# Router logits of five token groups moved from TensorE to VectorE, in a one-core attention, MLP and mixture-of-experts kernel

## The reference

```python
# attention: q, k, v (4, 8, 576, 64), mask: block of 64 of i >= block of j
x = attn_out.transpose(0, 2, 1, 3).reshape(2304, 512)
gate = 1.0 / (1.0 + np.exp(-(x @ w_gate)))          # w_gate, w_val (512, 1536)
x = (gate * (x @ w_val)) @ w_out                    # w_out (1536, 512)
logits = x @ moe2_w_gate                            # (512, 8)
expert_idx = np.argmax(logits, axis=1)
probs = softmax(logits)                             # denominator + 1e-9
for e in range(8):                                  # w1 (8, 512, 1024), w2 (8, 1024, 512)
    mask = expert_idx == e
    out[mask] = probs[mask, e] * (np.maximum(x[mask] @ w1[e], 0) @ w2[e])
```

## Time and profile before

| | |
|---|---|
| median of 3 runs | 969.89 us (969.75 to 971.04) |
| the profiled execution | 971.46 us, its span from first to last instruction 969.7 us |
| mean granted TensorE clock | 0.987 of full speed |
| TensorE products busy | 914.7 us, 94% of the span |
| VectorE busy | 391.9 us, 40% |
| ScalarE (ACT) busy | 297.2 us, 31% |
| GpSimd (POOL) busy | 260.2 us, 27% |

### The profile page before, as it was taken

How to read it: one execution, slowest core, us unless ns; L and a number is a source line. 1 busy time by engine, 2 the same in 40 slices (tenths; PEclk the granted TensorE clock), 3 DMA queues, 4 the chain that set the end, 5 groups by cost and what they waited for, 6 DMA issues and landing times.

```text
span 969.7 us, 15847 instructions
## 1 busy us (share of the span) xinstructions
PE 914.7 (94%) x5402; PEld 759.7 (78%) x5403; DVE 391.9 (40%) x851; ACT 297.2 (31%) x657; POOL 260.2 (27%) x253
## 2 busy tenths in 40 slices
PE   7988998999999999999999999999887999989995
PEld 3544554589999999999999999999766888878884
DVE  5766776731211321340241153145543345362241
ACT  4554554532221212112122111223132334361140
POOL 4122335421111111111111111122233435462251
PEclk9999999999999999999999999999999999999998
DMA  4545455422200100000010001111045246282130
GB/s 140 158 146 156 155 187 157 138 97 70 73 33 1 33 1 33 4 30 33 1 34 32 1 1 67 44 44 66 33 151 184 98 161 208 80 271 110 43 130 27
DMA packets 45545, 83.18 MB, mean 86 GB/s; under 512 B 6831, under 2 KB 19119, under 8 KB 45488
## 3 DMA queue, kind: packets, MB, share of 16 engines
q1 hardware_dynamic: 39728, 67.21, 21.1%
q0 software_dynamic: 3360, 10.49, 3.2%
q10 hardware_dynamic: 2400, 4.72, 1.3%
HBM read 68.17 MB, written 14.75 MB: 86 GB/s over the span
## 4 chain that ended last, share of the span: by engine, by line
PE 80%; DMA 7%; issue 4%; DVE 3%; POOL 2%; ACT 1%; SPq 1%; POOLq 0%; DVEq 0%; ACTq 0%
PE bank L1388 22%; PE bank L1390 22%; PE bank L1389 22%; DMA rinv_scratch<-rinv 3%; PE bank L1360 3%; PE bank L1321 3%; PE bank L1333 3%; DMA rwide<-rinv_scratch 2%; PE bank L1542 2%; PE bank L1450 2%; POOL w1l L441 1%; DVE nmax L976 1%; PE bank L1441 1%; PE bank L1510 1%; DMA stage<-in_we 1%
## 5 line engine op out<-in xcount | busy, mean ns | idle before, releaser
L1388 PE MATMUL bank<-xh,w1h 128*128 128x384 f32 x576 | 195.3, 339 | 0.0
L1390 PE MATMUL bank<-xh,w1l 128*128 128x384 f32 x576 | 193.0, 335 | 0.0
L1389 PE MATMUL bank<-xl,w1h 128*128 128x384 f32 x576 | 192.8, 335 | 0.0
L686 POOL TENSOR_TENSOR hl<-hraw,hh 128x384 fp32r<-128x384 f32 x72 | 77.6, 1077 | 399.7 <-ACT hh L829 399.7
L1134 DVE TENSOR_TENSOR hraw<-sig,bank 128x384 f32<-128x384 f32 x72 | 39.9, 554 | 269.8 <-ACT sig L873 234.6
L873 ACT ACTIVATE sig<-bank 128x384 f32<-128x384 f32 x72 | 35.4, 492 | 270.3 <-PE bank L1390 270.2
L1388 PEld LDWEIGHTS bank<-xh,w1h 128*128 128x128 f32 x576 | 108.2, 188 | 2.1
L1389 PEld LDWEIGHTS bank<-xl,w1h 128*128 128x128 f32 x576 | 108.2, 188 | 1.4
L1390 PEld LDWEIGHTS bank<-xh,w1l 128*128 128x128 f32 x576 | 108.1, 188 | 0.0
L800 ACT ACTIVATE prob<-bank,nmax 128x576 f32<-128x576 f32 (+2 forms) x144 | 76.0, 529 | 89.0 <-DVE nmax L976 87.9
L1390 PE MATMUL bank<-woh,hl 128*128 128x512 f32 x216 | 85.5, 396 | 0.0
(11 more groups left out here) (202 smaller groups left out, 1370.6 us busy)
## 6 DMA issues: line engine op xcount, KB each, us to landing
stage<-in_we SPq DMA_DIRECT2D x48, 512.0 KB, 4.5
w1raw<-in_w SPq DMA_DIRECT2D x8, 768.0 KB, 4.7
kt<-in_kT SPq DMA_DIRECT2D x16, 288.0 KB, 3.3
qt<-in_qT SPq DMA_DIRECT2D x16, 288.0 KB, 4.1
rwide<-rinv_scratch SPq DMA_DIRECT2D x32, 144.0 KB, 2.9
xt_scratch<-xo SPq DMA_DIRECT2D x16, 288.0 KB, 2.2
xraw<-xt_scratch SPq DMA_DIRECT2D x6, 768.0 KB, 4.6
y_scratch<-yrow ACTq DMA_DIRECT2D x6, 768.0 KB, 3.5
```

Of the source, the lines that this page charges most:

```text
L686: pool.tensor_tensor(hl[:, f % 2, :], hraw[:, f % 2, :], hh[:, f % 2, :].bitcast(F32), ALU.subtract).then_inc(h_low, 1)
L1388: pe.matmul(out_, wh, ah, start=first, stop=False, skip_group_check=True)
L1389: pe.matmul(out_, wh, al, start=False, stop=False, skip_group_check=True)
L1390: return pe.matmul(out_, wl, ah, start=False, stop=last, skip_group_check=True)
```

## The change

The logits of groups 0 to 4 are computed on VectorE: one `tensor_tensor_reduce` for each tile and expert multiplies the 512 values of a row of y with a column of the router's weights and sums them. The weights are spread over all partitions once (`wrb`, 2 MB, the eight experts side by side for each input). They stand in steps 0 to 7, three in each; in the last group 4, 4, 8 and 8 in steps 0 to 3. `routes`, `ranks`, `slots` with `spread`, and `table` follow in steps 8 to 11 (last group: 4 to 7), and the table is added at the next group's step 0. Group 5's own logits stay with TensorE. The ranks take two products instead of six, and the table holds only token numbers (144 columns).

The gates are no longer in the table: a small DMA stores each group's gates as column 513 of `y_dram`, so that a gathered row brings its gate, which GpSimd copies to `wcols` ahead of the next gather.

There is one x buffer: ACT and VectorE split the next group's x in four chunks behind the last `up` of a group, and the last two downs are no longer interleaved with ups of the next. `sig` is gone; the sigmoid is written to `hraw`. The y copies move from step 2 to step 0. The first expert's weights use the four stages of the others, and the steps of their splits are set in tables.

```diff
-    y_dram = nc.dram_tensor("y_scratch", (N, D), F32, kind="Internal").ap()
+    y_dram = nc.dram_tensor("y_scratch", (N, D + 1), F32, kind="Internal").ap()
...
+        def route_steps(G):
+            if G == G_LAST:
+                return [0, 4, 8, 16, 24], 4, 5, 6, 7
+            return [3 * f for f in range(9)], 8, 9, 10, 11
+
+        ROWS0_STEP = 9
+        HIGH_STEP = {6: [0], 7: [1, 2], 8: [3], 9: [4, 5], 10: [6, 7]}
+        LOW_V_STEP = {7: [0], 8: [2], 10: [4, 5], 11: [6]}
+        LOW_POOL_STEP = {8: [1], 9: [3], 11: [7]}
...
+            sp.dma_start(wrb[:].rearrange("p d e -> p (d e)"),
+                         wr.rearrange("(a d) e -> a (d e)", a=1).to_broadcast([P, D * E])).then_inc(wrb_loaded, 16)
+
+            def gate_store(G):
+
+                sp.wait_ge(gates_done, G + 1)
+                sp.dma_start(y_dram[G * GT:(G + 1) * GT, D:D + 1].rearrange("(m p) a -> p m a", p=P),
+                             gate[:].unsqueeze(2), allow_slow_non_contiguous=True).then_inc(gate_stored, 16)
+
             for G in range(2, NG):
                 xload(G, NPAIR)
+                gate_store(G - 2)
...
-                    if isinstance(l, int) and l == 0 and k == 3:
-                        low_wait(sp, l, 0)
+                    if isinstance(l, int) and l == 0 and k == 4:
+                        gate_store(G_LAST - 1)
                     if k >= 4:
-                        low_wait(sp, l, k - 3 if isinstance(l, int) and l == 0 else k - 4)
+                        low_wait(sp, l, k - 4)
...
             sp.wait_ge(first_known, 1)
-            sp.wait_ge(wo_low, FC)
-            sp.wait_ge(x_low, NG)
-            sp.wait_ge(gv_done, FC * G_LAST)
+            sp.wait_ge(lg_out, GM * G_LAST)
             load(0)
+            gate_store(G_LAST)
...
+                    pool.wait_ge(yg_loaded, 16 * t)
+                    pool.tensor_copy(wcols[:, bass.ds(t, 1)], yg[:, D:D + 1]).then_inc(gcol_done, 1)
...
+            def logits_of(G, lo, hi):
+
+                for n in range(lo, hi):
+                    m, e = n // E, n % E
+                    i = GM * G + m
+                    if e == 0:
+                        dve.wait_ge(y_out, i + 1)
+                    steps_done = GM * E * G + n
+                    if steps_done >= 2:
+                        dve.wait_ge(lg_step, steps_done - 1)
+                    junk = yT[:].rearrange("p c n -> p (c n)") if n % 2 else bank[3][:, 1, :]
+                    dve.tensor_tensor_reduce(junk, yrow[:, m, :], wrb[:, :, e], 1.0, 0.0, ALU.mult, ALU.add,
+                                             logits[:, i, e:e + 1]).then_inc(lg_step, 1)
+                    if e == E - 1:
+                        dve.wait_ge(lg_step, steps_done + 1)
+                        dve.sem_inc(lg_out, 1)
...
+                if G != G_LAST:
+                    xhigh(G + 1, [0])
+                hhigh(FC * G + FC - 1, 1)
+                if G != G_LAST:
+                    xhigh(G + 1, range(1, C))
...
-                pe.matmul(rank_psum, ltri_r[:], hot, start=True, stop=False, skip_group_check=True)
-                pe.matmul(rank_psum[:, E:], ones_r[:], hot[:, 0:(GM - 1) * E], start=False, stop=False,
+                pe.matmul(rank_psum, ones_r[:], hots[:, 0:GM + 1, :].rearrange("p m e -> p (m e)"), start=True, stop=False,
                           skip_group_check=True)
-                pe.matmul(rank_psum[:, 2 * E:], ones_r[:], hot[:, 0:E], start=False, stop=True, skip_group_check=True)
+                pe.matmul(rank_psum[:, 0:GM * E].rearrange("p (m e) -> p m e", e=E), ltri_r[:], oneh, start=False, stop=True,
+                          skip_group_check=True).then_inc(ranks_done, 1)
...
                     if f >= 2:
                         down(G, f - 2)
-                    elif not first:
-                        down(G - 1, FC - 2 + f)
...
+                    if not first and f == route_steps(G)[2]:
+                        ranks(G - 1)
+                    if not first and f == route_steps(G)[4]:
+                        table(G - 1)
                     if G == G_LAST and f == ROWS0_STEP:
-                        pe.wait_ge(base_done, G)
+                        pe.wait_ge(table_added, G)
                         turn_rows(0, True)
...
+                down(G, FC - 2)
+                down(G, FC - 1)
```

More of the change, by code:

```diff
@@ L118, in bass_attention_ffn_moe @@
         scol = sb(ctx, "scol", [P, 1], U32)
-        wcol = sb(ctx, "wcol", [P, 1])
-        yg = sb(ctx, "yg", [P, D])
+        wcols = sb(ctx, "wcols", [P, NTAB])
+        sc = ExitStack()
+        ltri = sb(sc, "ltri", [P, P])
+        ones = sb(sc, "ones", [P, P])
+        sc.close()
+        yg = sb(ctx, "yg", [P, D + 1])
         s12 = ExitStack()
@@ L165, in bass_attention_ffn_moe @@
         sx.close()
[L168 to L177, removed]
         sg = ExitStack()
         sb(sg, "over_x", [P, 3 * C * GT])
[L180 to L183, removed]
+        sb(sg, "over_hraw", [P, 2 * GT])
+        yT2 = sb(sg, "yT2", [P, C, P])
+        sb(sg, "over_gates", [P, 4 * GT - C * P + 2 * FC * D])
+        tab = sb(sg, "tab", [P, NCOL])
+        ag = sb(sg, "ag", [P, GM, NCOL], F32R)
+        b1h = sb(sg, "b1h", [P, GM, P], F32R)
+        assert (GM + 1) * NCOL + GM * P <= 2 * D
         sg.close()
@@ L227, in bass_attention_ffn_moe @@
         s3.close()
+        sb(s4, "over_tables", [P, 2 * FC * D - 2 * HC * D + 2 * D])
+        stage = [sb(s4, f"stage{i}", [P, F2]) for i in range(4)]
+        assert 4 * F2 == D * E and HC * P == F2
         s4.close()
@@ L405, in bass_attention_ffn_moe, with stage_at @@
         o_psum = bank[3][:, 0, :]
-        def stage_at(l, k):
-            return stage_first[k % 3][:] if isinstance(l, int) and l == 0 else stage[k % 4][:]
+        def stage_at(k):
+            return stage[k % 4][:]
         def low_wait(eng, l, k):
@@ L475, in bass_attention_ffn_moe @@
         for G in range(NG):
[L476 to L482, removed]
+            SHIFTED.append(n + 2)
+            ONEHOT.append(n + ROUTE_OPS)
+            n += ROUTE_OPS + SLOT_OPS + SPREAD_OPS + (GATE_OPS if G == G_LAST else 0)
+            TABLE.append(n)
+            n += GATE_OPS + 1 + (FIRST_OPS + ROWS_OPS if G == G_FIRST else 0)
         block = ctx.enter_context(nc.Block())
@@ L741, in _ @@
             pool.wait_ge(y_stored, 16 * NG)
+            pool.wait_ge(gate_stored, 16 * NG)
             gather(1)
@@ L871, in group @@
                     if not (first and f < 2):
-                        act.wait_ge(hraw_done, n - 1)
-                    act.activation(sig[:, f % 2, :], gv_psum(f)[0], ACT.Sigmoid).then_inc(sig_done, 1)
+                        act.wait_ge(h_high, n - 1)
+                        act.wait_ge(h_low, n - 1)
+                    act.activation(hraw[:, f % 2, :], gv_psum(f)[0], ACT.Sigmoid).then_inc(sig_done, 1)
                     if first:
@@ L1130, in group @@
                     dve.wait_ge(sig_done, n + 1)
-                    if not (first and f < 2):
-                        dve.wait_ge(h_high, n - 1)
-                        dve.wait_ge(h_low, n - 1)
-                    dve.tensor_tensor(hraw[:, f % 2, :], sig[:, f % 2, :], val_ps, ALU.mult).then_inc(hraw_done, 1)
+                    dve.tensor_tensor(hraw[:, f % 2, :], hraw[:, f % 2, :], val_ps, ALU.mult).then_inc(hraw_done, 1)
                     if first and f == 0:
@@ L1168, in _ @@
             for G in range(NG):
-                group(G, G % 2)
-            weights_low(dve, 0, 0, [k for k in LOW_V if k + EW_STEP + 1 >= FC], ew_low_v)
+                group(G)
             for m in range(GM):
-                yT_evac(GM * (NG - 1) + m, m, last=True)
+                yT_evac(GM * G_LAST + m, m)
             for m in range(GM):
-                lg_evac(GM * (NG - 1) + m, m, last=True)
+                lg_evac(GM * G_LAST + m, m)
             routes(G_LAST)
@@ L1579, in _ @@
             pe.wait_ge(exp_done, NB * NPAIR)
-            up(0, 0, 1)
+            up(0, 1)
             for G in range(NG):
-                group(G, G % 2)
-            down(NG - 1, FC - 2)
-            down(NG - 1, FC - 1)
-            i = GM * (NG - 1)
+                group(G)
             for m in range(GM):
-                turn_y(i + m, m, last=True)
+                turn_y(GM * G_LAST + m, m)
             for m in range(GM):
-                router(i + m, m, last=True)
+                router(m)
             expert_up(0, 0, 0)
             turn_hidden(0)
-            table_last()
+            table(G_LAST)
             expert_down(0, 0, 1)
```

338 lines of the change are left out of this document (137 added, 201 removed).

## The result

In the comparison behind the prediction the changed kernel took 955.32 us (median, 953.58 to 957.25) and the kernel before 970.46 on the same chip: a ratio of 0.984 with a 95% interval of 0.981 to 0.987, or -15.1 us. The forecast was 951.0 with a range of 941 to 961 and 0.92 for faster. The profiled execution has a span of 955.5 us against 969.7, at a mean granted clock of 0.976 against 0.987. So about a fifth of the forecast gain is missing, and most of this part is about where it went.

The account below looks back on a forecast made before the run. TensorE was taken to bound the kernel. From a span of 969.7 us, -27.4 (TensorE's stream), +8.2 (last group), +0.8 (first expert's weights), +0.1 (group 4's end) and -0.8 (tail) gave 950.6, forecast as 951, range 941 to 961.

Parts of the forecast that it names:

- TensorE's stream, -27.4: Groups 0 to 4: removing transposes, router products and their wait from TensorE saves 27.4 us, 26.1 at the other bound.
- The product, 1.05 us: Each new VectorE product of 512 elements, second operand at a 32-byte step, takes 1.05 us; bounds 0.63 and 1.6.
- The slope of L955: Existing VectorE operation reading one SBUF operand at nine floats' step: 1.94 ns an element, used to price the new product.
- contiguous rival: The 32-byte step costs nothing (0.63 us a product), so VectorE is no limit in the last group: 942.6 us; chance 0.24.
- Hidden in groups 1 to 4, and group ends: Products hide under TensorE in groups 1 to 4; splitting the next x at group ends costs nothing, 0.1 in group 4.
- rival of open group ends: At five group ends hl(11) and the x differences delay each other, up 0 waits 1.3 us: 957.5 us; chance 0.10.
- slower one: Products from 1.61 us make groups 1 to 4 wait too: 969.4 us at 1.65, 975 at 1.7; chance 0.06.
- The last group, +8.2: Last group: VectorE needs 36.0 us before the ranks, TensorE 29.3; a 6.7 us stall plus 1.5 for clock adds 8.2.
- The clock term: Last group, after the stall: three microseconds at half the clock (1.2 GHz) cost 1.5 us.
- First expert's weights, +0.8: Last group: late splits of the first expert's weights delay hl(10), so down 10 waits; 0.4 to 2.2 us, taken as 0.8.
- The tail, -0.8: After the last down: fewer rank products and earlier hrow save 1.0, extra gate copies cost 0.25; net -0.8, bounds 0 and -1.6.
- The sum: Whole kernel: 969.7 - 27.4 + 8.2 + 0.8 + 0.1 - 0.8 = 950.6 us of span, a change of -19.1.

Follow-up runs that it names:

- the other layout: Changed kernel with the router's weights laid out expert by expert, so each product reads 512 neighbouring floats: 945.03 us, 0.971 of the kernel before.
- the run with 21 tiles: Changed kernel with group 4's 24 products over only 256 of 512 values, so its tokens go to other experts: 956.57 us, 0.984 of the kernel before.
- the weights in pairs: Changed kernel with the router's weights in pairs of experts, read at a step of two floats instead of eight: 946.48 us, 0.973 of the kernel before.
- the ranks one step later: Changed kernel with ranks, slots and table of the last group in steps 6, 7, 8 instead of 5, 6, 7: 952.11 us, 0.979 of the kernel before.
- the second trace of the changed kernel: The changed kernel run again without any edit, as base beside another experiment: 955.43 us, 0.982 of the kernel before.

## Why the prediction came out as it did

**TensorE's stream, -27.4.** Right. Groups 1 to 3 give 81.2 - 75.65 = 5.55 us each, where 5.45 were forecast (27.4 is five times 5.47, before rounding); group 4 gives 0.5 less for its end, see below, and the fifth sits in the last group.

**The product, 1.05 us.** Right in kind and a little small: 1.09 from start to start. The slope of L955, at a step of nine floats, did carry over to eight. The Trainium skill (VectorE: DVE Perf Modes, Mode 1×) gives fp32 one result a cycle, odd strides included. Beyond a step of two floats the measurement differs from that, and it decides: 683 ns at two, 1,117 at eight. The contiguous rival was a right picture of another kernel: forecast at 942.6, built with the other layout it took 945.0.

**Hidden in groups 1 to 4, and group ends.** Right. No up waits for x or hraw in them; group 4's last step brings hl(11) late, and the sigmoids of step 0 of groups 4 and 5 are 76.18 us apart instead of 75.65: it cost 0.5, where 0.1 was forecast. The rival of open group ends and the slower one fall with this.

**The last group, +8.2.** The place and the mechanism were right (TensorE idle first at up 5, then at the ranks, then at half the clock); the size was short. VectorE's sum was 37.0 us where 36.0 were forecast. Hardly any of that is the product's price: the 24 products and the hl in their midst took 28.35 us, where 25.2 + 3.0 were forecast, since each of the three hl cost 0.73 to 0.85 us instead of 1.0 (0.85 = 1.94 - 1.09), which made up for most of the 0.04 of each product. The excess lies beside them: the table and first_rows with the gap behind them took 2.9 us instead of 2.4, and the five hraw with the gaps ahead of them 3.0 instead of 2.6. TensorE would have been there at 29.0 instead of 29.3: 8.0 us late instead of 6.7. The clock term was 1.5, and is 10.4 - 8.0 = 2.4. I had taken three microseconds at the low clock, the length of the stretch of the tail; behind the ranks it was 5.0 us in the first trace (from 620.45 to about 625.4) and 6.4 in the second. Together 10.4: this term is 2.2 too small.

**First expert's weights, +0.8.** The chain went as written down, link by link. GpSimd's rows:

```profile
652.01 1.02 POOL L689 TENSOR_TENSOR hl<-hraw,hh 128x384 fp32r<-128x384 f32 x1 [5.66 <-ACT hh L826]
652.98 2.42 POOL L436 TENSOR_TENSOR w1l<-stage,w1h 128x1024 fp32r<-128x1024 f32 x1
660.66 1.01 POOL L689 TENSOR_TENSOR hl<-hraw,hh 128x384 fp32r<-128x384 f32 x1 [5.26 <-ACT hh L826]
```

Chunk 3's difference follows hl(9), chunk 7 is in flight for 3.55 us behind it, and hl(10) comes last; down 10 starts at 661.81, 0.65 us behind the product ahead of it instead of 0.23, so it cost 0.4. The landing of 3.6 was the right one to take; my 0.8 lay between that and 4.5.

**The tail, -0.8.** This is the step that failed, by 3.6 us: from the last down's end to the end of the span it took 289.5 us, against 286.7 before. Of it 1.1 lie ahead of the first hrow (13.35 from the end of the last down instead of 12.2), and the rest in the steps behind it, where the clock was at 0.50 for 21.4 us in sum, against 13.8 before (7.6 us more at half the clock account for up to 3.8, and only 1.7 are lost there: what gave the others back isn't shown). One of these falls, from 847 on, has no counterpart before: turn_hidden's eight products take 1.94 us there instead of 1.06. The edits did what was forecast: both engines' hrow start together at 679.38, where VectorE was 0.7 behind the earlier trace rows. What I held fixed was the clock. From Y to H the table has three values for the changed code: 9.3 us without a fall, 10.9 or 11.0 with 3.4 us at 0.50, 12.5 with 6.8 us. The kernel before needed 11.4 with 3.4 us. So at an equal clock ACT's hrow comes 0.5 earlier, where 0.4 was forecast for the ranks, and VectorE's, which was 0.7 behind it before and no longer is, 1.2 earlier, where 1.0 was forecast; and each 3.4 us at 0.50 cost 1.6. Behind H it goes on: from Y to the end the table gives 283.7 to 289.0, with the kernel before, in one execution, in the midst (298.9 for the run with 21 tiles is left aside). The step failed in what it left out, not in what it counted: the clock moves this stretch by more than the edits do, in either direction.

**The sum.** From the forecast span of 950.6 to 955.5: last group's stall and clock +2.2, weights -0.4, group 4's end +0.4, tail +3.6, groups 1 to 4 -0.4, and the attention phase, whose code is the same, -0.5. That is all of the 4.9. The errors of +6.2 and -1.3 partly cancel, and the profiled execution was the longest of the four (957.25), so some of the tail's 3.6 may belong to it alone.

**Left open.** Why the clock falls once, twice or not at all in the tail of otherwise equal executions isn't settled. In the runs here a fall in the last group did not decide it: with the weights in pairs nothing waited there, and it fell all the same, from 660.3 to 663.7. Whether less time at the low clock behind the ranks can be had without taking the wait away was not tried.

## What to carry to other kernels

Before a loop moves to VectorE, look at the distance in bytes between neighbours of each operand: the layout that was natural for the matrix product (experts side by side) made every product take 1.09 us from start to start instead of 0.61, and passing the same numbers in another order was worth 10 us, two thirds of what the whole change gave. Work hidden in a steady stage is hidden only there: the last group, where the same work is squeezed into half the steps, needs a sum of its own, from one fixed event to the next, and the later of two such sums decides, however the waits ahead of it are cut. Where TensorE waits, add time at the low clock behind it: here a wait of 1.5 us passed without, and those of 1.9 us and more did not. And keep a few microseconds of range for the clock in any stage of short dependent products, where it fell without such a wait.

## What the runs showed of the hardware

The price of the distance between neighbours rises within a few bytes and then stays: 0.68 us at 4 and 8 bytes, 0.85 at 12, and 1.06 to 1.12 from 16 to 64 bytes for the reducing product; plain products, with SBUF or PSUM beside it, cost up to 0.05 more at each. I had expected 16 bytes to be cheaper than 32. And a wait of 2.0 us at up 5, behind a stretch in which TensorE had been busy at the full clock, was followed by products 0.32 us apart instead of 0.17, at a granted clock of 0.50. With the ranks one step later, waits of 2.1 and 1.9 us had the same behind them. In the second trace of the changed kernel a wait of 1.5 us at up 5 passed with the clock at 1.00:

```profile
604.00:606.00 2.00, 0.82 (x4) 0.35 (x2) 1.85 (x5) 0.00 (x0) 0.00 (x0) 1.00 0.00 0
606.00:608.00 2.00, 1.68 (x9) 1.68 (x10) 2.00 (x4) 0.91 (x2) 1.10 (x1) 1.00 0.00 0
608.00:610.00 2.00, 2.00 (x14) 2.00 (x13) 2.00 (x3) 0.00 (x0) 0.25 (x1) 1.00 0.00 0
```
